# A bulk weight load, an early value load and a reordered hand-over in a recurrence, gated MLP and mixture kernel

## The chip, the cores and the metric

One core of one Trainium2 chip runs the whole program in one launch. The metric is the device time of one execution in microseconds.

## The reference

Three layers follow each other, all in float32, for batch 4, sequence 768 and model width 320 (8 heads of 40):

1. A recurrence over the 768 time steps. Each of the 32 (batch, head) pairs keeps a 40 x 40 state; at step t the output is `r_t` times the state, and then the state is decayed by `w_t`, corrected by `(state @ a_t) b_t^T` and increased by `v_t k_t^T`.
2. A gated MLP: `h = relu(x @ w_in)` is split into halves `u` and `v`; `v` is normalised over its features, mixed over the sequence by `w_spatial` with a bias, multiplied by `u`, and projected by `w_out`.
3. A mixture of 8 experts, one per token, chosen by a gate or taken over from the token before.

## The kernel before, in words

The recurrence is done in 24 chunks of 32 steps. The loop over chunks stands in one `Block` in which each engine has its own instruction stream (`all_stages`); the streams are ordered by semaphores alone. TensorE runs the middle chunks as a hardware loop of sixteen small groups of 8 or 64 matmuls; ScalarE moves PSUM to SBUF (`drain`, line 1218), VectorE turns, adds and scans, GpSimd multiplies. SyncE issues the loads of a chunk: `kb` and `a` (two halves each), `v_tok` from `vt` (`load_v`, line 872), `v_own` from `vo` (line 875), `w`, `r` and, last in the chunk, `rg`. The load of `rg` is issued only after TensorE's `outputs` (line 1131) has used the buffer, and the drain of the transposed state (ScalarE, 104x640) waits for it; TensorE's `outputs_state` (line 1125) of the next chunk waits for that drain.

The ScalarE stream also issues the loads of the gated layer's weights on its own DMA queue, one a chunk: from chunk 1 the ten `gated.load` parts (six row tiles of the transposed `w_spatial`, 128 rows of 768 floats each, into `wspT`, then four parts of `w_in`), and behind them the ten `load_out` parts (`w_out` and the gate weights). The count of transfers, `self.transfers`, sets at which chunk `load_out` starts, and what GpSimd (`sum_weights`) and TensorE wait for before they use `wspT` and `win`. Nothing uses them before the recurrence ends. In the chunks with an even number the stream also stores the recurrence's result to `x_rows` in HBM.

The recurrence's result goes through HBM: SyncE reads it back as `xT` in tiles of 128 tokens, tile i with its own semaphore `x_tile[i]` (`load_tile`). The last tile, 5, can be read only after the last store, and that waits for the last `outputs` (line 1131, ps_B) and VectorE's product of it (`y_d`).

After the loop TensorE has a tail written out by hand: `unknowns` and `outputs_state` of the last chunk, `gated.values(0, 0)` (v of tiles 0 and 1 of batch 0), `turn_vu`, `gated.fold`, `gated.values(0, 2)`, `scores_r`, `outputs`, two `gated.gates`, `gated.values(0, 4)` (tiles 4 and 5) and so on. A pair (line 199) makes two groups: for each of two tiles two matmuls of 128x128 by 512 columns (line 206, four records each in the trace), and then a short one for the rest of the features of each (line 210). `between` is called between the first and the second of the groups. In it the kernel puts the small group `scores_r` (line 1114, ps_D), whose product VectorE masks (line 1398, `rvu`); `outputs` needs `rvu`. The x tile of the second group is waited for behind `between`.

At the start of the span the SyncE stream loads w, kb and a of chunk 0 and w of chunk 1. The load of `v_tok` of chunk 0 comes later, behind kb and a of chunk 1. VectorE reads it first in the second pass of TensorE's loop (line 1365).

Of the kernel before, what the change touches and what calls it, by code (L numbers as in the profile page):

```python
# [15 lines left out]
P = 128  # L16
BATCH, HEADS, SEQ, HD = 4, 8, 768, 40
DM = HEADS * HD
TILES = SEQ // P
# [3 lines left out]
D_HALF = D_FF // 2  # L23
# [8 lines left out]
NK = len(KCH)  # L32
# [43 lines left out]
class Gated:  # L76
# [4 lines left out]
    def __init__(self, nc, ctx, room, side, banks, x_rows, w_in, w_spatial, b_spatial, w_out, w_gate, w_local):  # L81
        def sem(name):
            return ctx.enter_context(nc.semaphore(name))

        self.sources = (w_in, w_spatial, b_spatial, w_out, w_gate, w_local)
        self.x_rows = x_rows
        low = Carver(room, EARLY * EXPERT_FLOATS, FIRST_END)
        self.v, vs, self.bsp = low("v", TILES, D_HALF), low("vs", 2, TH), low("bsp", SEQ)
        sb = Carver(room, FIRST_END, (EXPERTS - 1) * EXPERT_FLOATS)
        self.xT, self.win = sb("xT", NK, SEQ), sb("win", NK, D_FF)  # L90
        sb = Carver(room, (EARLY + 2) * EXPERT_FLOATS, (EXPERTS - 1) * EXPERT_FLOATS)
        self.wspT = sb("wspT", TILES, SEQ)
        sb = Carver(room, (EXPERTS - 1) * EXPERT_FLOATS, ROOM)
        self.wout, self.g, self.rows = sb("wout", ND, ROW), sb("g", ND, SEQ), side.rows
        self.stats, self.mv = sb("stats", TILES, 6), sb("mv", TILES, 2)
        self.sd, self.rs, self.half_sd, self.var = (sb(n, TILES) for n in ("sd", "rs", "half_sd", "var"))
        self.w_parts, self.v_parts = self.parts(self.wspT, TH), self.parts(self.v, D_HALF // 2)
        sb = Carver(side.hT.rearrange("p a f n -> p (a f n)"), 0, 2 * E_FF)
        w_top, more = sb("w_top", ST, TH), sb("more", 2, TH)
        self.upper_right, self.lower_left, self.first, self.second = vs[:, 0], vs[:, 1], more[:, 0], more[:, 1]  # L100
        sb = Carver(ctx.enter_context(nc.sbuf_tensor("sums", [P, ST * (TH + D_HALF)], F32)), 0, ST * (TH + D_HALF))
        w_bottom, v_late, v_early = sb("w_bottom", ST, TH), sb("v_late", ST, D_HALF // 2), sb("v_early", ST, D_HALF // 2)
        sb = Carver(side.w1_own.rearrange("p k f -> p (k f)"), 0, (NK - 1) * E_FF)
        w_both, v_both = sb("w_both", ST, TH), sb("v_both", ST, D_HALF // 2)
        self.w_sums, self.v_sums = (w_top, w_bottom, w_both), (v_early, v_late, v_both)
        A, B, D, G, E = banks
        self.pair_banks = {"GE": (G[:, :], E.rearrange("p a i t -> p (a i t)")), "B": (B[:, 0], B[:, 1]),
                           "D": (D[:, 0], D[:, 1])}
        self.vs_bank, self.o_bank = (D[:, 0], D[:, 1], A[:, 1]), (B[:, 0], B[:, 1])
        self.transfers = TILES + 1 + NK  # L110
        self.loaded, self.out_loaded, self.biased = sem("gated_loaded"), sem("out_loaded"), sem("biased")
        self.x_tile, self.x_full = [sem(f"x_tile{i}") for i in range(TILES)], sem("x_full")
        self.h_made, self.h_out = sem("h_made"), sem("h_out")
        self.vs_made, self.vs_out = sem("vs_made"), sem("vs_out")
        self.o_made, self.o_out = sem("o_made"), sem("o_out")
        self.stat, self.rooted, self.normed = sem("stat"), sem("rooted"), sem("normed")
        self.w_summed, self.v_summed, self.gated = sem("w_summed"), sem("v_summed"), (sem("gated0"), sem("gated1"))
# [4 lines left out]

    def load(self, eng, part):
        w_in, w_spatial, b_spatial, w_out, w_gate, w_local = self.sources
        pairs = [(self.wspT[:, t, :], w_spatial[t * P:(t + 1) * P, :]) for t in range(TILES)]
        pairs += [(self.win[0:n, k, :], w_in[lo:lo + n, :]) for k, (lo, n) in enumerate(KCH)]
        pairs += [(self.win[REST:, NK - 1, :], w_in[DM - REST:, :])]
        dst, src = pairs[part]
        eng.dma_start(dst, src).then_inc(self.loaded, 16)
# [82 lines left out]

    def values(self, pe, b, i, between=None):

        if b == 0:
            pe.wait_ge(self.x_tile[i], 16 * (NK + 1))
        if b >= 1 and i == 0:
            pe.wait_ge(self.x_full, 16 * (NK + 1) * b)

        def second():  # L220
            if between:
                between()
            if b == 0:
                pe.wait_ge(self.x_tile[i + 1], 16 * (NK + 1))

        self.pair(pe, self.v_at(b, i), D_HALF,
                  lambda g, k, rows: self.xT[rows, k, (i + g) * P:(i + g + 1) * P],
                  lambda g, k, rows: self.win[rows, k, D_HALF:], second)

    def gates(self, pe, b, j):  # L230

# [527 lines left out]
CHUNKS = SEQ // CH  # L759
# [7 lines left out]
def all_stages(nc, room, banks, inputs, x_rows, gated, side, routing, experts_w, experts):  # L767
# [3 lines left out]
    with ExitStack() as ctx:  # L771
# [83 lines left out]
        with nc.Block() as block:  # L855
            @block.sync
            def _(sp):
# [4 lines left out]
                def load_w(c):  # L862
                    halves(w_in[:, c % 2], wd, c, ld_w[c % 2], HALF if c < 2 else HD)
# [7 lines left out]
                def load_v(c):  # L871
                    sp.dma_start(v_tok.rearrange("p o n j e -> p (o n j e)"), vd[c]).then_inc(ld_v, 16)
# [6 lines left out]
                load_kb(0)  # L879
                load_a(0)  # L880
                load_w(1)
                for c in steps:
                    x, z = c + 1, c + 3
                    if c == -2:
                        sp.wait_ge(own_f, LEAD - 1)
                        load_own(0)
                    if c >= 0 and is_chunk(x):
                        sp.wait_ge(vu_done, x + LEAD)
                        load_v(x)
                    if c >= -2 and is_chunk(z):  # L890
                        sp.wait_ge(kbe_d, z)
                        load_kb(z)
                        sp.wait_ge(ae_d, z)
                        load_a(z)
                        if c == -2:
                            load_v(0)
                    if c >= -1 and is_chunk(c + 2):
                        sp.wait_ge(own_f, c + 1 + LEAD)
                        load_own(c + 2)
                    if is_chunk(c + 5):  # L900
                        sp.wait_ge(scan_f, c + 4)
                        sp.wait_ge(scan_b, c + 4)
                        load_w(c + 5)
                    if c == -1:
                        sp.wait_ge(gr_f, LEAD)
                        halves(cols(raw_rg), rgd, 0, ld_rg)
                        sp.wait_ge(rv_f, LEAD)
                        halves(cols(raw_r), rd, 0, ld_r)
                    if c >= 0 and is_chunk(x):
                        sp.wait_ge(rv_f, x + LEAD)  # L910
                        halves(cols(raw_r), rd, x, ld_r)
                        sp.wait_ge(yy_f, x + LEAD)
                        halves(cols(raw_rg), rgd, x, ld_rg)
                    if c >= 5 and c % 4 == 1:
                        for stored in y_st:
                            sp.wait_ge(stored, 8 * (c - 1))
                        gated.load_tile(sp, c // 4 - 1)
# [106 lines left out]
            def _(pe):  # L1024
# [84 lines left out]
                def scores_r(now):  # L1109
                    pe.wait_ge(vu_d_done, now)  # L1110
                    pe.sem_inc(passed, 1)
                    for o, n, mp, j in pairs():
                        m = 4 * o + n
                        mm = pe.matmul(D[rows(mp), j, m * CH:(m + 1) * CH], vu_d[rows(j), m, mp, :],  # L1114
                                       raw_r[rows(j), m, mp, :], start=True, stop=True)
                    mm.then_inc(rv_f, 1)
# [11 lines left out]
                def outputs(now):  # L1128
                    for o, n, mp, j in pairs():
                        m = 4 * o + n  # L1130
                        mm = pe.matmul(B[used(j), mp, m * CH:(m + 1) * CH], kb_tok[rows(mp), m, j, :],  # L1131
                                       rvu[rows(mp), j, m, :], start=False, stop=True, skip_group_check=True)
                    mm.then_inc(yy_f, 1)
# [41 lines left out]
                now = CHUNKS + LEAD  # L1175
# [5 lines left out]
                pe.wait_ge(vu_done, now)  # L1181
                turn_vu(now)
                gated.fold(pe, woutT, wgl, A[:, 1].rearrange("p (d n) -> p d n", n=P), folded)
                gated.values(pe, 0, 2, lambda: scores_r(now))
                pe.wait_ge(kt_d, CHUNKS)
                pe.wait_ge(rvu_d, now)
                outputs(now)
                gated.gates(pe, 0, 0)
                pe.wait_ge(y_d, CHUNKS + LEAD)
                gated.gates(pe, 0, 2)  # L1190
# [605 lines left out]
```

## Time and profile before

| | |
|---|---|
| three runs | 934.94, 935.22, 937.93 us; median 935.22 |
| the profiled execution | 934.94 us, span 933.2 us |
| granted TensorE clock | 0.995 over the span |
| TensorE busy (matmul) | 917.0 us, 98% |
| VectorE, ScalarE, GpSimd busy | 51%, 27%, 27% |
| DMA | 86.01 MB, mean 92 GB/s |

The span lies within the execution's own time; 1.7 us lie outside it. The recurrence fills the span up to 347 us, the gated layer and routing run to about 630 us, the experts to the end. A transfer's "us to landing" counts from its issue. In the chain of waits "issue" is time in which an engine waited for nothing that the profile shows.

### The profile page before, as it was taken

What the parts mean: (1) busy time and instruction counts of PE and PEld (TensorE: products, weight loads), DVE (VectorE), ACT (ScalarE), POOL (GpSimd) and SP (SyncE); (2) the same over time, 40 slices, a digit from 0 to 9 for tenths busy, and PEclk for the clock granted to TensorE, in tenths of its full rate; (3) what the DMA queues carried; (4) which work ended last, traced back from release to release, by engine and by line L of the source; (5) the groups of instructions that cost most, each with busy time, mean ns of one, the idle gap of its engine ahead of it and who ended that gap; (6) DMA issues with size and microseconds to landing.
All of it is one profiled execution on the core that took longest, in us unless ns stands there. A gap on an engine that the chain in (4) does not pass through costs nothing.

```text
span 933.2 us, 54057 instructions
## 1 busy us (share of the span) xinstructions
PE 917.0 (98%) x24653; PEld 712.9 (76%) x24654; DVE 477.5 (51%) x1026; ACT 250.4 (27%) x527; POOL 256.0 (27%) x231
## 2 busy tenths in 40 slices
PE   7999999999999999999999999999999999999997
PEld 6899999999999985545555545568888888888885
DVE  5478777877777643745455455463352222222230
ACT  0244444444444432102112112112212121212120
POOL 6354555456544551000020020020350111111011
PEclk9899999999999999999999999999999999999999
DMA  4235554654454321940110110339221010101000
GB/s 118 70 124 167 161 161 150 169 152 131 119 155 130 104 67 44 337 160 1 51 43 1 51 43 0 106 91 327 71 93 37 29 42 28 28 25 35 29 30 4
DMA packets 61477, 86.01 MB, mean 92 GB/s; under 512 B 22786, under 2 KB 41038, under 8 KB 61424
## 3 DMA queue, kind: packets, MB, share of 16 engines
q1 hardware_dynamic: 37232, 63.30, 22.0%
q10 hardware_dynamic: 21168, 13.32, 5.3%
q0 software_dynamic: 3024, 8.72, 2.6%
q8 instruction: 28, 0.46, 0.2%
q14 instruction: 25, 0.20, 0.1%
HBM read 72.47 MB, written 14.45 MB: 93 GB/s over the span
## 4 chain that ended last, share of the span: by engine, by line
PE 98%; issue 1%; DMA 0%; ACT 0%; DVE 0%; POOL 0%; SPq 0%; DVEq 0%; POOLq 0%; ACTq 0%
PE ps_D L1589 14%; PE ps_D L288 8%; PE ps_G L1571 6%; PE ps_E L1571 6%; PE ps_B L300 6%; PE ps_E L1079 5%; PE ps_A L288 4%; PE ps_B L206 3%; PE ps_G L1578 3%; PE ps_D L1114 3%; PE ps_E L1077 3%; PE ps_D L1051 3%; PE ps_G L206 3%; PE ps_E L206 3%; PE ps_D L1153 2%; PE ps_A L1056 2%
## 5 line engine op out<-in xcount | busy, mean ns | idle before, releaser
L1589 PE MATMUL ps_D<-room,hT 128*128 x496 | 138.8, 433 | 0.0
L1589 PEld LDWEIGHTS ps_D<-room,hT 128*128 128x128 f32 x496 | 91.9, 190 | 34.7
L1532 POOL DMA_INDIRECT out<-y,token x31 | 34.8, 1123 | 254.9 <-DVE y L1697 184.7
L644 POOL DMA_INDIRECT sorted_rows<-rows,slot x24 | 23.9, 996 | 237.6 <-DVE slot L636 231.5
L1697 DVE TENSOR_SCALAR y<-ps_D,x_in 128x320 f32<-128x320 f32 x31 | 17.0, 550 | 125.5 <-PE ps_D L1589 125.5
L1680 DVE COPY w_own<-room 128x1024 f32 x62 | 44.3, 720 | 63.1 <-PE ps_G L1571 34.5
L1633 ACT ACTIVATE hT<-ps_G 128x512 f32<-128x512 f32 x31 | 18.5, 598 | 216.2 <-PE ps_E L1578 216.2
L1329 DVE STREAM_TRANSPOSE room<-room 128x256 f32<-128x256 f32 x96 | 42.3, 441 | 49.0 <-ACT room L1218 49.0
L1571 PEld LDWEIGHTS ps_G<-xTt,w_own 128*128 128x128 f32 x496 | 60.0, 192 | 5.3 <-issue 0.8
L1571 PE MATMUL ps_G<-xTt,w_own 128*128 128x128 f32 x496 | 60.6, 275 | 0.6 <-ACT hT L1633 0.6
L1571 PE MATMUL ps_E<-xTt,w_own 128*128 128x128 f32 x496 | 60.4, 275 | 0.0
L1571 PEld LDWEIGHTS ps_E<-xTt,w_own 128*128 128x128 f32 x496 | 57.9, 192 | 0.0
L1003 POOL TENSOR_TENSOR room<-room 128x640 f32<-128x640 f32 x23 | 46.4, 2019 | 30.3 <-DVE room L1377 30.3
L300 PE MATMUL ps_B<-room 128*128 128x329 f32 x192 | 54.6, 441 | 0.0
L1218 ACT ACTIVATE room<-ps_E 128x256 f32<-128x256 f32 (+1 forms) x96 | 35.0, 364 | 67.6 <-PE ps_E L1079 36.4
L979 POOL TENSOR_TENSOR room<-room 128x1024 f32<-128x1024 f32 x24 | 52.2, 2175 | 1.9
L300 PEld LDWEIGHTS ps_B<-room 128*128 128x128 f32 x192 | 36.0, 190 | 18.4 <-issue 2.3
L1014 POOL TENSOR_TENSOR room<-room 128x256 f32<-128x256 f32 x24 | 15.7, 656 | 124.0 <-DVE room L1421 124.0
L1218 ACT ACTIVATE room<-room 128x512 f32<-128x512 f32 (+2 forms) x72 | 40.2, 558 | 34.5 <-PE ps_B L1131 31.2
L1079 PE MATMUL ps_E<-room 32*32 32x48 f32 (+1 forms) x3200 | 47.8, 205 | 0.2 <-issue 0.2
L1079 PEld LDWEIGHTS ps_E<-room 32*32 32x32 f32 x3200 | 40.5, 104 | 5.7 <-issue 4.7
L1218 ACT ACTIVATE room<-ps_D 128x1024 f32<-128x1024 f32 x24 | 24.6, 1026 | 48.6 <-PE ps_D L1051 48.6
(256 smaller groups left out, 1773.1 us busy)
## 6 DMA issues: line engine op xcount, KB each, us to landing
room<-in_moe_w SPq DMA_DIRECT2D x8, 1280.0 KB, 13.5
room<-in_moe_w SPq DMA_DIRECT2D x8, 1024.0 KB, 11.0
room<-in_vt SPq DMA_DIRECT2D x24, 320.0 KB, 3.8
room<-in_kb SPq DMA_DIRECT2D x46, 160.0 KB
x_in<-sorted_rows ACTq DMA_DIRECT2D x27, 161.0 KB, 2.2
room<-in_vo SPq DMA_DIRECT2D x24, 160.0 KB, 4.1
room<-in_rg SPq DMA_DIRECT2D x48, 80.0 KB
room<-in_r SPq DMA_DIRECT2D x48, 80.0 KB
```

The lines of the kernel that those rows point to most:

```text
L206: pe.matmul(self.bank_of(n + g)[:, 0:width], left(g, k, slice(0, P)), right(g, k, slice(0, P)), start=(k == 0), stop=False, skip_group_che ...
L288: mm = pe.matmul(self.vs_bank[n % 3][:, 0:TH], left[:, s, c * P:(c + 1) * P], right[:, s, :], start=(s == 0), stop=(s == ST - 1))
L300: mm = pe.matmul(self.o_bank[n % 2][:, 0:ROW], self.g[:, d, i * P:(i + 1) * P], self.wout[:, d, :], start=(d == 0), stop=(d == ND - 1))
L979: pool.tensor_tensor(kb_end.rearrange("p m n k t -> p (m n) k t"), raw_kb[:, :, :, :], later[:, :, None, :].broadcast_to([P, GROUPS, 2, CH ...
L1003: pool.tensor_tensor(faded.rearrange("p m n e -> p (m n) e")[:, :, 0:HD], stateT.rearrange("p m n e -> p (m n) e"), whole[:, x % 4, :, Non ...
L1079: mm = pe.matmul(E[q, :, i, kept], pw[q, i, :], powers[q, l - 2:ROUNDS - 1:ROUNDS - l, i, kept], start=True, stop=True)
L1218: act.activation(out, in_, ACT.Copy).then_inc(done, 1)
L1329: dve.transpose(pw.rearrange("p i t -> p (i t)"), (powers[:, l - 1] if l else qi[:, 0]).rearrange("p i t -> p (i t)")).then_inc(flip_d[l], 1)
L1532: pool.indirect_dma_start(out=self.out[:, :], out_offset=bass.IndirectOffsetOnAxis(ap=side.token[:, u:u + 1], axis=0), in_=side.y[:, u % 2 ...
L1571: mm = pe.matmul(self.ps_h[half][:, f, :], side.w1_own[:, k, col:col + P], x[:, k, :], start=(f == 0 and k == 0), stop=False, skip_group_c ...
L1589: mm = pe.matmul(self.ps_y[:, u % 2], side.hT[:, u % 2, f, :], self.weights.w2[:, bass.ds(e, 1), f, :], start=(f == 0), stop=(f == self.NF ...
L1680: dve.tensor_copy(side.w1_own[:, :, cols], w1.w1[:, bass.ds(e, 1), :, cols].rearrange("p o k f -> p (o k) f")).then_inc(self.w1_in, 1)
```

## The change

There are four edits.

- `w_spatial` is loaded by one DMA of 768 rows of 3072 bytes in place of six of 128 rows. `self.transfers` falls from 10 to 5, so that the `w_in` parts and the `load_out` parts each come five chunks earlier.
- `load_v(0)` is issued before the chunk loop of SyncE, right behind w of chunk 1.
- `values` for batch 0 waits for both x tiles of its pair before its first group.
- In TensorE's tail `scores_r` is called before `gated.values(0, 2)`, and `outputs`, with its waits for `kt_d` and `rvu_d`, is called between the two groups of that pair.

```diff
-        self.transfers = TILES + 1 + NK
+        self.transfers = 2 + NK
...
-        pairs = [(self.wspT[:, t, :], w_spatial[t * P:(t + 1) * P, :]) for t in range(TILES)]
+        pairs = [(self.wspT[:, :, :], w_spatial.rearrange("(t p) s -> p t s", p=P))]
...
     def values(self, pe, b, i, between=None):
 
-        if b == 0:
-            pe.wait_ge(self.x_tile[i], 16 * (NK + 1))
+        for t in (i, i + 1):
+            if b == 0:
+                pe.wait_ge(self.x_tile[t], 16 * (NK + 1))
         if b >= 1 and i == 0:
             pe.wait_ge(self.x_full, 16 * (NK + 1) * b)
-
-        def second():
-            if between:
-                between()
-            if b == 0:
-                pe.wait_ge(self.x_tile[i + 1], 16 * (NK + 1))
-
         self.pair(pe, self.v_at(b, i), D_HALF,
                   lambda g, k, rows: self.xT[rows, k, (i + g) * P:(i + g + 1) * P],
-                  lambda g, k, rows: self.win[rows, k, D_HALF:], second)
+                  lambda g, k, rows: self.win[rows, k, D_HALF:], between)
...
                 load_w(1)
+                load_v(0)
                 for c in steps:
...
-                        if c == -2:
-                            load_v(0)
...
                 gated.fold(pe, woutT, wgl, A[:, 1].rearrange("p (d n) -> p d n", n=P), folded)
-                gated.values(pe, 0, 2, lambda: scores_r(now))
-                pe.wait_ge(kt_d, CHUNKS)
-                pe.wait_ge(rvu_d, now)
-                outputs(now)
+                scores_r(now)
+
+                def final_outputs():
+                    pe.wait_ge(kt_d, CHUNKS)
+                    pe.wait_ge(rvu_d, now)
+                    outputs(now)
+
+                gated.values(pe, 0, 2, final_outputs)
                 gated.gates(pe, 0, 0)
```

## Rows read from the trace of the kernel before

**Rows 1.** The page's part 4, shares of the chain of work that ended last.

```profile
...
PE 98%; issue 1%; DMA 0%; ACT 0%; DVE 0%; POOL 0%; SPq 0%; DVEq 0%; POOLq 0%; ACTq 0%
...
```

**Rows 2.** The chain of waits, start of the span: start us, us, what.

```profile
...
5.25 0.29 issue
...
8.25 2.09 issue
...
17.61 0.25 issue
...
20.49 1.45 issue
...
23.64 1.65 issue
...
26.92 1.56 PE ps_B L1056 x8
...
41.28 0.85 PE ps_B L1056 x8
...
```

**Rows 3.** The same chain where the recurrence ends; no other wait stands from 30 us on.

```profile
...
343.51 1.95 DMA room<-in_rg
...
```

**Rows 4.** Busy time by stretch; the last columns are PEclk, DMA share, GB/s.

```profile
...
6.00:8.00 2.00, 2.00 (x124) 2.00 (x125) 1.82 (x4) 0.00 (x0) 1.74 (x13) 1.00 0.90 233
8.00:10.00 2.00, 0.25 (x12) 0.10 (x5) 1.87 (x4) 0.00 (x0) 1.87 (x7) 1.00 0.19 53
17.00:20.00 3.00, 2.75 (x142) 2.33 (x137) 1.11 (x1) 0.71 (x1) 0.00 (x0) 1.00 0.77 227
22.00:25.00 3.00, 1.64 (x127) 1.43 (x128) 0.00 (x0) 0.00 (x0) 2.92 (x3) 0.71 0.02 5
58.00:66.00 8.00, 7.95 (x511) 7.29 (x503) 6.88 (x14) 3.06 (x6) 2.42 (x2) 1.00 0.60 196
59.00:61.00 2.00, 2.00 (x137) 1.78 (x135) 1.62 (x3) 1.27 (x2) 1.49 (x1) 1.00 0.96 369
...
```

**Rows 5.** DMA issues by line, from the DMA view: KB each, us to landing.

```profile
...
room<-in_vt SPq DMA_DIRECT2D x24, 320.0 KB, 3.8
...
room<-in_moe_w_spatial ACTq DMA_DIRECT2D x6, 384.0 KB, 4.5
...
room<-x_rows SPq DMA_DIRECT2D x12, 32.0 KB, 1.9
...
```

**Rows 6.** The timeline of ACT, 57 to 60 us: start us, us, engine, line.

```profile
...
57.15 0.40 ACTq L129 DMA_DIRECT2D room<-in_moe_w_spatial  x1
59.61 1.03 ACT L1218 ACTIVATE room<-ps_D 128x1024 f32<-128x1024 f32 x1 [2.08 <-PE ps_D L1051]
...
```

**Rows 7.** Every issue of the expert loads on SP: duration ns min/median/max.

```profile
...
L416 SPq DMA_DIRECT2D room<-in_moe_w x32: 390/596/7383, 370.1 to 639.9; - x32
...
```

**Rows 8.** The timeline of all engines around one load of in_rg.

```profile
...
66.28 0.67 SPq L860 DMA_DIRECT2D room<-in_rg  x2
...
68.78 0.70 ACT L1218 ACTIVATE room<-ps_B 104x640 f32<-104x640 f32 x1 [0.72 <-DMA room<-in_rg]
...
70.19 0.81 PE L1125 MATMUL ps_B<-room 64*40 64x32 f32 x64
...
```

**Rows 9.** The timeline of all engines where the recurrence ends.

```profile
...
358.06 1.14 PE L1114 MATMUL ps_D<-room 64*64 64x32 f32 x64
...
359.27 0.69 DVE L1398 TENSOR_TENSOR room<-ps_D,room 128x512 f32<-128x512 f32 x1 [12.09 <-PE ps_D L1114]
...
362.10 0.81 PE L1131 MATMUL ps_B<-room 64*40 64x32 f32 x64
...
368.86 0.60 SPq L154 DMA_DIRECT2D room<-x_rows  x1
...
370.09 1.98 PE L206 MATMUL ps_G<-room 128*128 128x512 f32 x4
...
```

## The prediction

> **What bounds the kernel now.** I read the shares of the chain of waits first: 98% of what ended last is TensorE's matmuls, 1% is "issue", and all DMA together rounds to nothing [rows 1]. So a transfer made better pays only where TensorE was waiting, and one made worse costs only where its slack runs out. Four places are touched: the startup, chunk 1 of the recurrence, the chunks that lose or shift a ScalarE issue, and the tail of the recurrence. For each I looked for TensorE's waits in the chain, and then for the slack of the transfer next to it. The reader is to see five "issue" gaps in the first 26 us [rows 2]. From there to the end of the recurrence the chain has one other wait, for `rg` of the last chunk [rows 3], which nothing here moves.
>
> **The startup.** TensorE's gaps of 0.29, 2.09, 0.25, 1.45 and 1.65 us [rows 2] come with no semaphore behind them. Between them it started some 126 pairs of weight load and matmul by the counts in the chain, or twice that where a gap is absent: it waits for instructions, one block at a time. From gap end to gap end: 5.54 to 10.34 is 4.80 us, 17.86 to 21.94 is 4.08 us, 21.94 to 25.29 is 3.35 us. The first had a DMA share of 0.90 over its first part and 0.19 over the rest, the second 0.77 in front, the third 0.02 [rows 4]. So a block takes about 3.35 us on quiet DMA engines and 1.45 and 0.73 us more beside data.
>
> The edit moves 320 KB of `vt` [rows 5], 0.33 MB, out of the second interval into the first. At 233 and 227 GB/s [rows 4] that is 1.4 us of traffic either way. In the first interval some 2.9 us of traffic (5.5 to 8.4) cost 1.45, so 1.4 more cost 1.45 x 1.4 / 2.9 = +0.7 us; bounds 0 (another engine's queue holds the load) and +1.4 (all of it in front of the block). In the second some 3.4 us of traffic cost 0.73, so taking 1.4 away gives -0.3 us; bounds 0 and -1.45, the whole gap. TensorE is the only engine of the chain here, so the sum stands as +0.4 us. SyncE itself waits until 9.9 us for VectorE's scan before its next load, so one more issue there is free; `kb`, `a` and both `w` are ahead of `vt` in the queue. VectorE wants `vt` only in the second pass of the loop, after 28 us, and it landed by 22, so an earlier landing gives nothing.
>
> The clock adds a bound. It was granted at 0.71 over 22 to 25 us [rows 4], that is a part of the stretch at the lower of its levels, 1.2 GHz, after TensorE had stood idle for 3.1 us in two gaps; the group at 26.92 us took 1.56 us where the same took 0.85 us one chunk on [rows 2]. With a smaller second gap this drop may not come: -0.7 us on this group and, I estimate, as much again on its four neighbours, -1.4. I take 0, since the third gap, the longer one, stays.
>
> The Trainium skill (Runtime: NRT & Kernel Launch, Instruction fetch mechanics) says that instructions come in blocks of 256 through a DMA queue of the engine itself and that this is mostly hidden. The block size agrees with the 126 pairs; "mostly hidden" doesn't hold for these gaps, and by it the sum would be 0 instead of +0.4.
>
> **One DMA for w_spatial.** Six issues of 384 KB [rows 5] become one of 2304 KB at 57.15 us, where the first stands today [rows 6]. What is removed is worth nothing: each issue takes 0.40 us, within 2.08 us in which ScalarE idles ahead of its drain at 59.61 [rows 6]. No chunk with such an issue shows a wait in the chain [rows 3]. The new issue generates 768 rows instead of 128. The expert loads, up to 1024 rows, took 0.39 us at the least, 0.60 in the median and 7.38 where their queue was full [rows 7]. Here ScalarE's queue is empty, so I take 0.6, hidden; it shows beyond 0.4 + 1.7 = 2.1 us, and a full queue would cost 7.4 - 2.1 = 5.3.
>
> What is added is a burst. In 58 to 66 us the engines moved 8 x 196 = 1.57 MB [rows 4], of that 0.39 of `w_spatial`. With 2.36 in its place it is 3.54 MB; at 369 GB/s, the mean of 59 to 61 [rows 4], that is 9.6 us, to 67.6. The one load with little slack is `rg`, issued at 66.28 and landed at 68.78, where ScalarE's 0.70 us drain starts. `outputs_state` starts at 70.19 [rows 8], so `rg` may be 0.7 us later. If the two queues share evenly, `rg`'s 0.16 MB waits for as much of the burst: 0.16/0.369 = 0.4 us, hidden. If `rg` gets nothing until the burst ends it is 67.6 - 66.28 = 1.3 us late, and 0.6 us show; at only 227 GB/s [rows 4] the burst would last to 73.6, and 7.3 - 0.7 = 6.6 us would show. Not below 0: no wait of TensorE stands here to be gained. I take +0.2, near the even share, which is the nearer row because the peak rates were measured at this very place. The chunk's other loads are needed a chunk or more later. It happens once. The later parts come five chunks earlier into chunks that had parts of the same size; nobody reads them before 347 us: 0.
>
> The Trainium skill (DMA: Bandwidth & Descriptors, Queues, rings and completion order) lets an engine alternate between queues by packets of about 9 to 17 descriptors. No row here shows such a packet; with it `rg` would wait for one or two packets more per engine, an estimate between the even share and the 0.6 above, so it speaks mildly against the edit.
>
> **The tail.** The same matmuls run in another order, and a small group still stands between large ones as often: 0 of work. `scores_r` needs ScalarE's drain of `turn_vu`, which ends under the fold. After `scores_r` VectorE needs from 359.20 to 359.96 (359.27 + 0.69) for `rvu` [rows 9], 0.76 us; the first group of the pair, 1.9 us, lies over it, and without that cover 0.76 would show. `outputs` then starts at about 356.2 + 1.1 + 1.9 = 359.2 instead of 362.10, so `y_d`, the store and tile 5 come 2.9 us earlier. Tile 5's last load, issued at 368.86 and 1.9 us on its way [rows 5, 9], landed at 370.8; it was needed behind the first group begun at 370.09, and is now needed before it. At 370.8 - 2.9 = 367.9 it is in time by 2.2 us (1.1 before). So the earlier wait costs nothing; alone, without the earlier `outputs`, it would cost 0.7. TensorE never waited for tile 5, so nothing is gained. The relus of tiles 2 and 3 and the copy of the fold come about 0.8 us later, behind the moved `outputs`; GpSimd's last sum hangs on them, and TensorE reads it more than 20 us on. SyncE's expert loads start 3 us earlier, 260 us before their use.
>
> **Sum.** Startup +0.4, burst +0.2, tail 0: 934.94 + 0.6 = 935.5 against the profiled execution's own time. That execution is 0.28 below the median of the runs shown, so I predict 935.8 for a median. About 0.3%, 2.8 us, is what a measurement of this kernel can tell from no change: from 932.4 to 938.0.
>
> **The rivals.**
> *Slower, through `rg`* (chance 0.08). The burst holds `rg` back until it is through, and runs slower than at its start. It decides past 0.3% when 3.54 MB last beyond 69.8 us, at under 300 GB/s. For it: the small-row loads of the startup reach only 227 to 233 GB/s. Against: 369 GB/s at this place. At 298, midway, the burst ends at 69.9, `rg` is 3.6 late, 2.9 show in place of 0.2: 938.5.
> *Faster, through the startup* (0.06). The early `vt` adds nothing to the first block, the second gap of 1.45 closes, and the clock isn't lowered: -1.45 - 1.4 in place of +0.4, so 935.8 - 3.25 = 932.5. For it: blocks are slower beside data. Against: the block of 3.35 us had none beside it and still left a gap.
> *The tile wait* (0.04). If `outputs` isn't earlier, since `rvu` or `kt_d` is late, tile 5 arrives at 370.8 and 0.7 us show: 936.5. Against: 1.1 us of cover over `rvu`.
> *The change doesn't do what it says.* The single load could be split over fewer engines and be slow, yet its reader is 280 us away; this is the case of the burst that ends late but lets `rg` through, with the forecast's time.
>
> **How the numbers follow.** My forecast holds 0.82; its own range is 933.7 (nothing on the first block, the second gap gone, no burst: -0.7 - 1.15 - 0.2) to 937.2 (startup +1.4, burst +0.6). The runs shown lie from 0.3 below their median to 2.7 above it, and the rivals stand at 932.5 and 938.5; that widens the range to 932.9 to 938.2. Faster by over 0.3%: 0.05, most of the faster rival. Slower: 0.07, most of the `rg` rival. The same: 0.88.
>
> **What would show it.** In the changed profile the gaps at 8.25 and 20.49 us should be about 2.8 and 1.2 us; if both are unchanged, instruction loads don't care for `vt`. At the one `w_spatial` issue ScalarE should spend about 0.6 us, and the next drain of `rg` start near 69.2 less any shift from the startup; a TensorE gap before line 1125 there is the rival. The DMA share should be near 1 from 59 to 67. `outputs` should stand inside the second pair, three microseconds earlier against the fold's end, tile 5 land before the third pair, and the stage from the fold to the first mix last as long as before. A difference of over 1 us behind the recurrence would mean that I missed a wait there.

## The result and the profile after

The changed kernel took 941.72 us in the median (939.70 to 943.29, 8 runs) where before took 936.64 (934.94 to 939.39, 8 runs) in the same rounds: a ratio of 1.0054, 95% interval 1.0039 to 1.0070. I had forecast 935.8 with 0.88 on no change; it is slower, by some 5 us. The profiled execution took 940.78 us with a span of 939.0 and a mean granted clock of 0.990; before's had 934.94, 933.2 and 0.995.

The page's part 4, the shares of the chain of waits after the change, answers to [rows 1]; DMA, which rounded to nothing, has a percent of its own now:

```profile
...
PE 97%; issue 1%; DMA 1%; ACT 0%; DVE 0%; POOL 0%; SPq 0%; DVEq 0%; POOLq 0%; ACTq 0%
...
```

The chain of waits in chunk 1 of the recurrence (start us, us, what) shows where that percent is:

```profile
...
65.95 5.32 DMA room<-in_rg
...
71.30 0.71 ACT room L1215
72.01 0.30 issue
72.31 0.81 PE ps_B L1118 x62
...
```

SyncE issues `rg` at 65.63 us, and it lands 5.6 us later, at 71.28; before it took 2.5 [rows 8]. ScalarE's drain follows at once, and TensorE's `outputs_state` (line 1118 now) 0.30 us behind the drain's end. The stretches (the last columns are PEclk, DMA share, GB/s) answer to [rows 4], the last one to the tail:

```profile
...
58.00:66.00 8.00, 7.95 (x518) 7.30 (x519) 7.11 (x14) 3.44 (x7) 2.33 (x2) 1.00 1.01 333
66.00:71.00 5.00, 3.61 (x230) 3.17 (x218) 2.28 (x5) 0.76 (x2) 3.60 (x3) 1.00 0.67 236
358.00:364.00 6.00, 6.00 (x74) 4.37 (x74) 0.69 (x1) 0.00 (x0) 0.00 (x0) 0.50 0.00 0
...
```

From 58 to 71 us the engines moved 8 x 333 + 5 x 236 = 3.84 MB, at a mean of 295 GB/s. The loads issued from 56 us up to and with `rg` hold 3.84 MB by their sizes, so `rg` lands when about all of it is through. The one `w_spatial` issue and its landing (duration ns, first and last start us; then us to landing), and the load of `vo` issued inside the burst, which took 2.8 us at this place before:

```profile
...
L129 ACTq DMA_DIRECT2D room<-in_moe_w_spatial x1: 454/454/454, 56.5 to 56.5; - x1
...
DMA to landing us min/median/max: 13.4/13.4/13.4
```

```profile
...
L869 SPq DMA_DIRECT2D room<-in_vo x1: 351/351/351, 60.4 to 60.4; - x1
...
DMA to landing us min/median/max: 7.7/7.7/7.7
```

So the burst is through at 69.9 us, not 67.6, and a load of 160 KB on the other queue takes 7.7 us beside it.

The second place is the tail. The chain there, from the fold on, answers to [rows 9]:

```profile
...
355.58 3.94 PE ps_A L167 x24
359.53 1.86 PE ps_D L1107 x64
361.39 3.51 PE ps_G L206 x4
364.90 0.74 PE ps_B L1124 x64
...
```

The fold took 3.94 us, `scores_r` 1.86 and the first group of the second pair 3.51, where before's chain has 3.24, 1.07 and 1.91. The granted clock was at 0.50 over 358 to 364 us, its lower level, 1.2 GHz; before it was at 1.00 there. The work is the same and nobody waits. Half the loss between the two profiles stands here; whether it belongs to the change is for the experiments (x2, b1).

The startup's gaps answer to [rows 2]:

```profile
...
7.39 2.16 issue
...
15.68 1.52 issue
...
19.83 0.90 issue
...
22.36 1.73 issue
...
```

Stage by stage, from the chains of both profiles: `outputs_state` of the third pass starts at 43.26 us instead of 43.91. From there to the first v group of the tail it takes 306.61 instead of 303.35, from there to the first mix 37.93 instead of 34.84, and the rest 551.20 instead of 551.10. I use these four stages below, and call the second "the recurrence" and the third "the tail".

### The profile page after: what moved, and what is told of

It reads as the page before. It is cut to its first block, busy times and chain, and to the rows that moved or that the text cites. A ratio compares the mean times of both kernels' runs of the same rounds, so it can differ in the third digit from the quotient of the medians.

```text
span 939.0 us, 54053 instructions
## 1 busy us (share of the span) xinstructions
PE 919.0 (98%) x24653; PEld 713.8 (76%) x24654; DVE 475.2 (51%) x1026; ACT 250.4 (27%) x527; POOL 255.7 (27%) x231
## 4 chain that ended last, share of the span: by engine, by line
PE 97%; issue 1%; DMA 1%; ACT 0%; DVE 0%; POOL 0%; SPq 0%; DVEq 0%; POOLq 0%; ACTq 0%
PE ps_D L1586 14%; PE ps_D L282 8%; PE ps_G L1568 6%; PE ps_E L1568 6%; PE ps_B L294 6%; PE ps_E L1072 5%; PE ps_A L282 4%; PE ps_B L206 3%; PE ps_G L1575 3%; PE ps_D L1107 3%; PE ps_D L1044 3%; PE ps_E L1070 3%; PE ps_G L206 3%; PE ps_E L206 2%; PE ps_D L1146 2%; PE ps_A L1049 2%
```

## The experiments

All are compared with the kernel before on the same chip. Where a time has a ratio, its interval is at 95%.

**x1_single_load**: the kernel before with the single load alone.

```diff
-        self.transfers = TILES + 1 + NK
+        self.transfers = 2 + NK
...
-        pairs = [(self.wspT[:, t, :], w_spatial[t * P:(t + 1) * P, :]) for t in range(TILES)]
+        pairs = [(self.wspT[:, :, :], w_spatial.rearrange("(t p) s -> p t s", p=P))]
```

> The kernel before with one part of the change alone: the single load of w_spatial. Theory (the burst holds back the load of rg of chunk 1): one wait of about 2.7 us for rg ahead of TensorE's outputs_state near 72 us, the w_spatial load landing some 13 us after its issue, and about 2.8 to 3.3 us more than before. Rival (rg is late only together with the early value load): no such wait, within 0.5 us of before.

Measured: 942.47 us (6 runs) against 937.02 (29), a ratio of 1.0060 (1.0044 to 1.0075). This one edit alone loses as much as the whole change. Its chain has the wait, and behind it something that the changed kernel's profile doesn't show:

```profile
...
66.09 5.53 DMA room<-in_rg
...
74.26 1.90 PE ps_D L1051 x8
76.16 1.38 PE ps_E L1079 x64
...
```

```profile
...
70.00:73.00 3.00, 0.39 (x41) 0.42 (x44) 0.00 (x0) 1.36 (x3) 0.00 (x0) 1.00 0.71 227
74.00:77.00 3.00, 3.00 (x63) 2.59 (x59) 1.99 (x2) 0.74 (x1) 1.86 (x2) 0.50 0.80 232
...
```

The turns on ps_D (line 1051) took 1.90 us and the level behind them 1.38; a chunk without a fall has 1.03 and 0.92. TensorE stood idle for 3 us, and 2 us after `rg` had landed the granted clock fell to 0.50 for 3.4 us. The recurrence took 308.51 us, 4.7 more than the second profile of before (b1, below) has. `outputs_state` started at 72.61, where two chunks of 13.18 us from 43.39 make 69.75: 2.9 us of it are the wait. The three groups behind it took 1.5 us more than in a chunk without a fall.

**a1_after, a2_after, b1_before**: both kernels again, unchanged, for more profiles.

> The changed kernel, unchanged, for a second profile. Theory (the wait for rg, 2.8 us, lets the clock fall behind it in part of the executions): rg lands about 1 us behind the burst, TensorE waits 2.5 to 3 us, and in about half of the profiles a stretch at 1.2 GHz follows between 70 and 80 us, worth 1.5 us. Rival (the rest of the loss is elsewhere): none here in any, and a difference of over 1 us from before in another stage.

> The changed kernel, unchanged, for a third profile; theory and rival as for the second.

> The kernel before, unchanged, for a second profile of it. Theory (TensorE's clock falls in the tail in most executions of either kernel, and the first profile of before is one of the few without): a stretch at 1.2 GHz between 350 and 370 us and 936 to 939 us. Rival: none, as in the first profile, and the fall belongs to the change.

Measured: 945.27 and 947.45 us for the changed kernel, 938.60 for before (one execution each), on a chip where before had a median of 939.70 over 17 runs. The chain of the second profile after the change:

```profile
...
67.42 5.93 DMA room<-in_rg
...
76.70 1.90 PE ps_D L1044 x8
78.60 1.46 PE ps_E L1072 x64
...
```

The clock was low for 6.8 us here, from just before `rg` landed, and for 3.4 us in a2. Over the four profiles that have the burst in its place the recurrence took 306.61 (no fall), 309.28, 308.77 and 308.51 us (falls of 6.8, 3.4 and 3.4 us), 308.3 in the mean. The two of before have 303.35 and 303.81. The fall goes with the wait in three of four. Counted from one `outputs_state` to the next, the wait alone took 2.7, 3.3, 3.2 and 2.9 us, and the next chunk 2.4, 1.6 and 1.6 us more than 13.18 where a fall came. In the nine profiles of this study without a wait of 2.5 us or more in chunk 1 the granted clock doesn't fall once between 40 and 340 us. In a2 the experts' part was 2.6 us longer than in a1, with a wait of 2.0 us for a turned x tile, up to 706.6 us, and a fall from 707 us behind it; only one profile has that, and why the tile was late stays unexplained.

The tail of before isn't free of falls either. Its second profile, where the first had 3.24, 1.91 and 1.07:

```profile
...
353.32 3.24 PE ps_A L167 x24
356.56 3.43 PE ps_G L206 x4
359.99 1.18 PE ps_D L1114 x64
...
```

The clock was low from 356 to 361 us and the tail took 36.46 us instead of 34.84. Of 14 profiles of all kernels of this study only the first of before has no fall in the tail. That profile, at 934.94 one of the fastest of all executions of before, is not the usual one.

**x2_tail_order**: the kernel before with the reordered tail alone.

```diff
-                gated.values(pe, 0, 2, lambda: scores_r(now))
-                pe.wait_ge(kt_d, CHUNKS)
-                pe.wait_ge(rvu_d, now)
-                outputs(now)
+                scores_r(now)
...
+                gated.values(pe, 0, 2, final_outputs)
```

> The kernel before with the reordered tail alone: scores_r ahead of the second pair, outputs inside it. Theory (the longer run of small groups, turn_vu, fold and scores_r, lets TensorE's granted clock fall in the tail): a stretch at 1.2 GHz near 355 to 365 us and 1 to 3 us more than before. Rival (the fall seen in the changed kernel depends only on when the tail comes, not on its order): no fall or one as often as before, and within 0.5 us of before.

Measured: 937.60 us (12 runs), ratio 1.0007 (0.9996 to 1.0017). The rival holds:

```profile
...
352.69 3.24 PE ps_A L167 x24
355.93 1.60 PE ps_D L1114 x64
357.53 2.98 PE ps_G L206 x4
...
```

The clock fell here too, but the tail took 36.43 us against 36.46 in before's second profile, with the old order. From the fold's end to `outputs` it was 4.6 us here and 7.6 there, so `outputs` does come 3.0 us earlier. The order costs nothing that can be measured.

**y1_six_loads**: the changed kernel with six loads again (the first diff reversed).

> The changed kernel with w_spatial in six loads again; everything else of the change stays. Theory (the single load is the whole loss, directly by the late rg and by the clock falls behind it): no wait for rg in chunk 1, and within 0.2% of before, so some 5 us less than the changed kernel. Rival (the reordered tail or the early value load costs too, as the two profiles suggest by the tail's 3.1 us): 2 to 3 us more than before.

Measured: 937.81 us (12 runs) against 936.89 (25), ratio 1.0007 (0.9995 to 1.0019). Taken from both sides, the single load is the loss: the other three edits together are worth between -0.5 and +1.8 us. The recurrence took 304.27 us with no wait in chunk 1; the tail had a fall of 6.8 us and took 37.92, as in the changed kernel.

**y3_late_issue**: the changed kernel, the single load issued later in the chunk.

```diff
-                    if 1 <= c <= gated.transfers:
+                    if 2 <= c <= gated.transfers:
                         gated.load(act, c - 1)
...
                         square(x, 3)
+                    if c == 1:
+                        gated.load(act, 0)
```

> The changed kernel, but the single load is issued some 5 us later in the same chunk, behind ScalarE's third square drain. Theory (rg does not land before the burst is through, whatever is left of it): the burst ends 5 us later, the wait for rg grows from 2.7 to about 7 us, and the kernel takes about 5 us more than the changed one, 946 to 948. Rival (the two queues share, and a load beside the burst takes about 5.5 us wherever the burst stands): the wait stays near 2.8 us and so does the time.

Measured: 946.16 us (6 runs), ratio 1.0090 (1.0072 to 1.0107). ScalarE's issue, and the wait in the chain:

```profile
...
64.03 0.45 ACTq L129 DMA_DIRECT2D room<-in_moe_w_spatial  x1
...
```

```profile
...
67.65 7.99 DMA room<-in_rg
...
```

The load landed after 11.0 us, at 75.0, and `rg` at 75.64, 8.3 us after its issue; 5.3 us of that showed (76.62 where two chunks from 44.94 make 71.30), and a fall of 6.8 us came with it; the recurrence took 311.80 us. It was issued 3.3 us behind the burst instead of 9.1, had the same 2.36 MB beside it and came 5.8 us late instead of 3.1. An even share for `rg` alone, my step, would have given the same delay in both. From 65 to 75.6 us the engines moved 3.32 MB, while the single load, `w`, `r` and `rg` hold 2.86: loads issued behind `rg` (`vt` at 71.34, `kb` at 71.73) took a part as well.

**w1_early_issue**: the changed kernel, the single load issued earlier, behind the drain that waits for the `rg` before.

```diff
-                    if 1 <= c <= gated.transfers:
+                    if 2 <= c <= gated.transfers:
...
                         drain(by_head(fadedT[0:LIVE]), by_half(B[0:LIVE]), fT_f, c + LEAD, fT_d)
+                    if c == 1:
+                        gated.load(act, 0)
```

> The changed kernel, but the single load is issued 0.8 to 1.4 us earlier in the chunk, right behind ScalarE's drain that waits for the rg before. Theory (rg lands when the burst is through): the wait shortens by as much as the issue moves, to some 1.7 us, and with it the clock falls behind it; 1 to 2.5 us less than the changed kernel, 939 to 941. Rival (a fixed delay per burst): 941 to 942 as the changed one.

Measured: 941.79 us (12 runs) against 939.70 (17) on the chip of a1, a2 and b1, ratio 1.0032 (1.0017 to 1.0048), where the changed kernel has 1.0054 (1.0039 to 1.0070); the intervals overlap, so that this is faster is likely and not shown by the times. The issue and the wait:

```profile
...
56.20 0.45 ACTq L129 DMA_DIRECT2D room<-in_moe_w_spatial  x1
...
```

```profile
...
67.11 3.85 DMA room<-in_rg
...
```

The issue stands 10.6 us ahead of `rg`'s, at 66.78, instead of 9.1. Of the wait 1.2 us showed (`outputs_state` at 71.94 where two chunks of 13.18 from 44.41 make 70.77) instead of 2.7 to 3.3, no fall followed in this profile, and the recurrence took 304.95 us. The burst itself landed at 67.6, 0.8 us behind `rg`'s issue; still `rg` took 4.2 us. What it stood behind by then was mostly no longer the burst but its own queue: `vo`, issued at 61.58, took 7.4 us, and `w` and `r` were issued before `rg` too. From 67 to 71 us the engines moved 4 x 160 = 0.64 MB, and `vo`, `w`, `r` and `rg` hold 0.66. So, by these numbers, not the burst alone holds `rg` back, but all that was issued earlier and is still open on either queue. No run moves `rg`, `vo`, `w` or `r` themselves, which would test this directly.

**y2_two_loads**: the kernel before with two loads of 1152 KB, one chunk apart.

```diff
+        self.transfers = 3 + NK
...
+        pairs = [(self.wspT[:, t:t + ST, :], w_spatial[t * P:(t + ST) * P, :].rearrange("(t p) s -> p t s", p=P))
+                 for t in (0, ST)]
```

> The kernel before with w_spatial in two loads of three row tiles, one chunk apart. Theory (what counts is whether a burst is still under way when rg is issued, 9 us later): 1.2 MB end before that, no wait for rg, same as before. Rival (any load larger than 384 KB delays rg, in proportion): two waits of about 1 us, 2 us more than before.

Measured: 938.64 us (11 runs) against 936.89, ratio 1.0018 (1.0006 to 1.0030). Neither theory holds. `rg` landed in time in both chunks, yet there is a loss, and ScalarE's timeline shows another one:

```profile
...
69.53 0.42 ACTq L130 DMA_DIRECT2D room<-in_moe_w_spatial  x1
69.99 2.92 ACTq L854 DMA_DIRECT2D x_rows<-room  x2
73.01 1.02 ACT L1219 ACTIVATE room<-ps_D 128x1024 f32<-128x1024 f32 x1 [3.10 <-issue]
...
```

In chunk 2 the store of `x_rows` is issued right behind the second load on the same queue. Issuing it took 2.92 us instead of 1.02, and the drain behind it began 3.10 us later than the instruction before it ended, so TensorE's group on line 1115 waited 0.75 us. The recurrence took 304.40 us, 0.6 more than in before's second profile; the median's loss is 1.7 us (0.6 to 2.8), so this wait may be only a part of it. That the second load makes the stores slow to issue is read from this one profile and not tested. Smaller bursts avoid the one wait and meet the other; six loads meet none.

**x4_tile_waits**: the kernel before, both x tiles waited for in front.

```diff
             pe.wait_ge(self.x_tile[i], 16 * (NK + 1))
+            pe.wait_ge(self.x_tile[i + 1], 16 * (NK + 1))
...
-                pe.wait_ge(self.x_tile[i + 1], 16 * (NK + 1))
```

> The kernel before, but both x tiles of a pair of batch 0 are waited for ahead of its first group. By the rows of before tile 5 lands at 370.8 us and the third pair starts at 370.09: 0.7 us more than before, as a gap ahead of the third pair. Rival: the tile has landed and nothing changes.

Measured: 938.94 us (12 runs), ratio 1.0015 (1.0000 to 1.0030). The gap ahead of the third pair is there:

```profile
...
375.62 1.03 issue
...
```

In this profile the early wait costs 1.0 us alone. Its tail took 39.09 us, with a fall of 6.8 us in it as well. In the changed kernel the earlier `outputs` pays for it: tile 5's last load is issued at 371.65 and the third pair starts at 375.86 without a wait.

**x3_early_v**: the kernel before with the early load of `v_tok` alone.

> The kernel before with load_v of chunk 0 issued behind w of chunk 1 alone. By the changed kernel's trace the second pass of the loop starts 0.65 us earlier: 0.65 us less than before. By the prediction's sum: 0.4 us more.

Measured: 936.70 us (12 runs) against 937.02 (29), ratio 0.9994 (0.9983 to 1.0005). Neither sign is shown. The gaps of its profile:

```profile
...
5.25 0.29 issue
...
7.36 3.04 issue
...
17.23 1.14 issue
...
21.00 1.17 issue
...
23.80 2.00 issue
...
```

Together they are 7.64 us, against 5.73 in before's first profile and 6.31 in the changed kernel's with the same early load. The third pass's `outputs_state` started at 43.94 us here; in the other profiles with the late load it stands at 43.10 to 45.41, and at 43.26 to 44.94 with the early one. Over all 14, seven of each, the means are 43.88 and 44.31: 0.4 us apart, within a scatter of 2.3, which can't tell such an edit.

**z1_fold_apart**: the kernel before with the fold moved between the first two pairs of gates, as an attempt to beat it.

```diff
-                gated.fold(pe, woutT, wgl, A[:, 1].rearrange("p (d n) -> p d n", n=P), folded)
...
                 gated.gates(pe, 0, 0)
+                gated.fold(pe, woutT, wgl, A[:, 1].rearrange("p (d n) -> p d n", n=P), folded)
```

> The kernel before with the fold (24 matmuls of 9 columns) moved from behind turn_vu to between the first two pairs of gates, so that TensorE's small groups of the tail no longer follow each other. Theory (the run of small groups lets the granted clock fall in the tail, in most executions and with either order): no fall between 345 and 375 us, the stage from the first v group to the first mix takes 34.8 us as in the profile of before, and 1 to 2 us less than before in the median. Rival (the fall comes from the wait for the last rg): it stays.

Measured: 941.52 us (8 runs), ratio 1.0041 (1.0025 to 1.0057). Both theories fall. The chain of the tail in two parts:

```profile
...
353.98 1.03 ACT room L1218
355.00 0.49 ACT room L307
...
355.63 1.96 PE ps_G L206 x4
...
```

```profile
...
365.99 3.79 PE ps_A L167 x24
369.78 5.42 PE ps_B L206 x8
...
```

The fold had covered ScalarE's drain and its relu of the ps_E bank, for which TensorE now waits 1.7 us. And the clock fell all the same, from 368 to 376 us, behind the fold alone, and over the longest pair. The fall isn't the wait for the last `rg`, which ends 20 us earlier, and not a run of several small groups either. But it moved with the fold, by some 12 us: in all 13 profiles that have a fall in the tail it begins 2.2 to 4.4 us behind the fold's start. So the fold is the suspect that is left; no run leaves it out, and the first profile of before has the fold and no fall. The tail took 40.05 us. No version of this study beats before.

## Why the prediction was wrong

*What bounds the kernel*: right. TensorE is the chain, and a transfer costs when its slack runs out. I also named `rg` of chunk 1 as the one with little slack. But it had 0.4 to 0.5 us of it, not 0.7: I left out the 0.3 us between the drain's end and `outputs_state`. After the change `rg` came 3.1 us late and 2.7 showed; in y3 5.8 and 5.3.

*One DMA, what is removed and the issue itself*: right. The issue took 0.45 us instead of 0.40, and no chunk became shorter.

*One DMA, the burst*: this is the step that failed. "If the two queues share evenly, `rg`'s 0.16 MB waits for as much of the burst: 0.16/0.369 = 0.4 us, hidden", and from it "I take +0.2". Three things were wrong with it. First, the share is decided earlier than at `rg`: while the burst is under way, `vo`, `w` and `r`, issued ahead of `rg` on its own queue, pile up in front of it (`vo` took 7.7 us instead of 2.8). Even with a fair share `rg` comes at the end of all of it: 3.84 MB were moved from 58 to 71 us, and it landed at 71.28. Second, the rate: I took 369 GB/s from the two best microseconds; over the 13 us of the burst it was 295. The rival of 0.08, deciding at under 300 GB/s, priced the wait at 2.9 us, and it was 2.7 to 3.3 in four profiles; that the price fits is in part luck, since it had `rg` 3.6 us late with a slack of 0.7 where the changed kernel's profile has 3.1 and 0.4. Third, the wait isn't the whole price. With TensorE idle for some 3 us its clock fell in three of four profiles, and the mean of the four recurrences is 308.3, 4.5 to 4.9 us over the two of before, out of a loss of 5.1 in the medians. I had read that very pattern in the startup, two gaps with the granted clock at 0.71 behind them [rows 4], and didn't carry it to the wait that I priced. With it the rival would have stood at about 940. Its threshold was off too: from 935.6 without the burst, 2.4 us shown reach 938.0, so it decides beyond 69.4 us, at under 311 GB/s, not beyond 69.8.

The Trainium skill (DMA: Bandwidth & Descriptors, Queues, rings and completion order) has the queues take turns by packets. Nothing here contradicts that: `vo` did get through inside the burst, in 7.7 us. The turns say how two queues share, not how long the queue is in front of one load; it was I who left that out.

*The tail*: the sum of 0 is right for order and waits together (ratio 1.0007, 0.9996 to 1.0017), and `outputs`, 2.9 us earlier by my step, does carry the tile wait, which alone costs 1.0 us (I had 0.7). The profiles of before and after differ by 3.1 us here by a clock fall that 13 of 14 profiles have, of both orders, and that happened to be absent in the one I worked from. What decides its length, 3.4 or 6.8 us, and its absence, stays open.

*The startup*: +0.4 is neither shown nor refuted (x3: -1.6 to +0.5 us). The two gaps that I had at 2.8 and 1.2 us came out at 2.16 and 0.90 in the changed kernel, and at 3.04 and 1.17 in x3; the gap between them, 0.25 before, was 1.52 and 1.14. The sum of the gaps varies by more between profiles than the step is worth.

*The base*: I added 0.28 us between profile and median. Over 54 runs on two chips before has a mean of 937.2 us, 2.3 above the profiled one. My range was too low by that as well.

## What to carry to other kernels

A merged load has to be judged by the tightest load issued while it is under way: add up every byte issued before that load on all queues and still open, divide by a rate held over the whole burst, and compare with its slack. Loads issued behind it can add to that, as in y3. Then price a TensorE wait of some 3 us with the clock fall that may come with it, here 1.6 to 2.4 us on top in three of four profiles. And a single profile of before is one draw: where clock falls of 3.4 us come and go, a difference of 3 us in a stage between two profiles needs a second profile before it has a cause.

## What the hardware showed that I had not expected

- A DMA issue on ScalarE behind a 1152 KB load on the same queue took 2.92 us instead of 1.02 for two stores (y2), although the load itself was issued in 0.42 us.
- TensorE's clock fell with the engine busy all the time. In z1 it stood at 0.50 from 369 to 375 us, while the end of the fold and the pair of gates behind it followed each other without a gap.
- Leaving out the last 15 us of the span, every fall in the 14 profiles took 3.4 us or twice that (by the granted clock per microsecond: 356.2 to 359.6 us in x2, 357.7 to 364.6 after the change).
- TensorE's gaps with no semaphore behind them in its first two passes (those of 0.2 us or more) come to 5.1 to 7.6 us in total, in a different split in most profiles.
